# Complex-decay attention and two gated layers on one core: attention work spread over five positions of a slot

## The chip, the cores and the metric

The kernel runs on one core of one Trainium2 chip. Time is device microseconds of a whole execution. The engines are TensorE (PE in the profile), VectorE (DVE), ScalarE (ACT), GpSimd (POOL) and SyncE (SP), which issues most DMAs. Each engine works through its own program in order and waits for the others by semaphores.

## The reference

Three computations follow one another. The first is attention by a recurrence with complex decays, for 4 batches, 8 heads, 768 steps and a head width of 48:

```python
mag = np.sqrt(a_re * a_re + a_im * a_im)
scale = np.minimum(mag, 0.999) / (mag + 1e-06)
a_re_n, a_im_n = (a_re * scale, a_im * scale)
for t in range(S):
    new_re = ar * S_re - ai * S_im
    new_im = ar * S_im + ai * S_re
    S_re, S_im = (new_re + kv, new_im)          # kv = k_t outer v_t
    y[:, :, t] = np.einsum('bhd,bhde->bhe', q[:, :, t], S_re)
```

Its output, as 3072 tokens of 384 numbers, goes through `g = h * clip(h + 3, 0, 6) / 6; g @ w_out` with `h = x @ w_in` (384 to 2048 and back), and then through a second layer of the same sizes with `g = max(h, 0) + alpha * min(h, 0)`. All in float32.

## The kernel before

Attention is cut into 24 chunks of 128 steps (`NCH`), six to a batch, all heads at once. A chunk's decays become a magnitude part (`t_fb`: forward and backward running products, by scans on VectorE) and a phase part (`t_phase`, then `t_frac`, the turn without its whole part, then `t_trig`, cosine and sine on ScalarE). `prod` is q and k times these. Eight DMAs from SP and four from ScalarE's queue (`stack`) lay `prod` out by head in `st`. On TensorE then come `score` (two banks of four heads, `gp` and `yp`), `turn_k` (k transposed), `outputs` (masked scores times v, plus the carried state) and `new_state` (k times v, in `gp`). VectorE masks the scores (`mask`) and makes the next carried state `s_pad` (`state`); ScalarE copies the transposed k (`copy_k`).

The feed-forward layers work on units of 384 tokens, three chunks each. Every float32 operand is split in a high part and a low part, and each product takes three matmuls (`three`). An item n is one block of 128 hidden columns of one unit; 16 items make a unit. `hidden(n)` is nine matmuls of 384 columns from `x_parts` into one of two `hp` banks, `output(n)` nine into `op`. Between them lie the gate on ScalarE (`gate_of`), its product on VectorE (`gate1`), the high part on ScalarE (`high`) and the low part on GpSimd (`low`). TensorE runs `output(n)` and then `hidden(n + 3)`; the other engines work two items ahead (`n + 2`). At the end of a unit ScalarE copies `op` to `out_sb` (`leave`), and the next unit's first `output` waits for that (`o_left`). The second layer runs after all of the first; its items have no attention beside them.

The order of everything is written out by hand. `places()` yields slots s = -3 to 24 with five positions (six where a slot has six items). In a slot s the code handles four chunks at different ages: c0 = the slot's own chunk (scores to state), c1 = the next (angle, phases, products, stack), c2 (magnitude, clip, inverse, ratios), c3 (squares). Slot 3 has no chunk of its own, so chunks from 3 on sit in slot c + 1. Slots 3 to 6 have 3, 4, 3 and 4 items, from slot 7 on 5, 5, 6 in turn. The first `hidden` stands in slot 2. At each position an engine does its part of the item and then its pieces of attention work, in this order in the kernel before:

- VectorE (lines 819 to 853): position 0 `mags(c2)`, `phases(c1)`, `fractions(c1)`, both `mask(c0)`; position 1 `forward`, `backward`, `products` of c1; position 2 `x_low`, `state` of c0, `clip`, `numerators` of c2; position 3 two of three `inverse(c2)`; position 4 the third and `ratios(c2)`. `ratios` ends with a clamp of the tangent to 1.5 either way (line 686).
- ScalarE (lines 588 to 618): position 0 `angle(c1)`, `copy_k`; position 1 `waves(c1)`, `copy_k`, `magnitude(c2)`; position 2 `x_high(c0)` and, behind `high`, the four DMA issues of `stack(c1)`; position 4 `squares(c3)`. A weight split (`split_w`, line 567, its low half on GpSimd, line 471) stands at the end of a position: three each in slots -2 to 1, four each in slots 2 to 4 (`W_SPLITS`). A split waits for its piece of `wa_raw` or `wb_raw`.
- SP (lines 379 to 399): at position 2 `stack(c1)` behind `prod_done`, `spread(c0)` behind `x_done` (six DMAs inside `x_parts`, which hidden(16u) needs for all three chunks of unit u), the loads of `a` and of q and k; at position 3 the load of v and of weights.
- TensorE (lines 1061 to 1080): position 0 `score(c0, 0)`, `turn_k`, the item's output, `score(c0, 1)`, the item's hidden, `turn_k`; position 1 the item, `outputs`, `new_state`.

`score(c, 0)` writes the bank `gp` and waits for `state_ready` of the chunk before, which reads `gp`.

## Time and profile before

| | us |
|---|---|
| median of three runs (1093.77 to 1096.41) | 1095.03 |
| the profiled execution | 1091.72 |
| its span, first to last instruction | 1089.9 |
| PE busy | 971.5 |
| DVE busy | 700.0 |
| ACT busy | 487.9 |
| POOL busy | 304.5 |
| mean granted clock of TensorE | 0.986 |

The profile page cuts the span into 40 slices and lists groups of instructions by line; the trace can be asked for stretches, waits and single instructions. A wait line says which engine and line sat idle, for whom, for how long in total, how often and the longest. Starts of instructions are microseconds from the start of the span.

### The profile page before, as it was taken

Reading aid. Unit: us, or ns where it says so; the run is one execution under the profiler, and the core shown is the slowest. Engines: PE = TensorE matmul, PEld = TensorE weight load, DVE = VectorE, ACT = ScalarE, POOL = GpSimd, SP = SyncE. Lnnn points to the kernel's source line nnn. Section 1 sums busy time; section 2 is a strip of 40 time slices with the busy share of each in tenths; the row PEclk is TensorE's granted clock in tenths of the full one; section 3 lists DMA queues with packets and bytes.
Section 4 is the critical chain, followed back from the end, with each engine's and each line's share of the span. In section 5 each row is a group of like instructions: output and inputs, shape, how many; then the busy total and the mean of one; then the engine's idle time right before and its main releaser. Section 6 shows DMA issues by size and latency. Waiting matters only on the chain.

```text
span 1089.9 us, 16711 instructions
## 1 busy us (share of the span) xinstructions
PE 971.5 (89%) x6178; PEld 952.6 (87%) x6178; DVE 700.0 (64%) x1234; ACT 487.9 (45%) x814; POOL 304.5 (28%) x291
## 2 busy tenths in 40 slices
PE   0156698699999999999999999999999999999998
PEld 0156687699998898989999999999999999999998
DVE  1884899799898898998989224553334344343432
ACT  2553766556766666667665345321212221221211
POOL 1222431122222222222221233333333333333332
PEclk9999899899999999999999999999999999999999
DMA  8353223333342332333323360101101010101000
GB/s 164 101 156 75 68 71 77 85 97 75 95 103 69 93 82 82 97 87 91 93 56 82 94 221 1 45 1 44 35 11 44 1 45 1 44 1 44 1 23 23
DMA packets 84803, 72.84 MB, mean 67 GB/s; under 512 B 34928, under 2 KB 80496, under 8 KB 84336
## 3 DMA queue, kind: packets, MB, share of 16 engines
q1 hardware_dynamic: 75120, 63.43, 21.3%
q10 hardware_dynamic: 9600, 8.33, 3.0%
q8 instruction: 49, 0.80, 0.3%
q14 instruction: 34, 0.28, 0.1%
HBM read 40.90 MB, written 9.44 MB: 46 GB/s over the span
## 4 chain that ended last, share of the span: by engine, by line
PE 55%; DVE 19%; ACT 8%; SPq 7%; issue 6%; DMA 4%; ACTq 1%; DVEq 0%
PE hp L1023 9%; PE op L1023 9%; PE hp L1025 9%; PE hp L1024 9%; PE op L1025 9%; PE op L1024 8%; SPq L358 3%; DVE t_phase L693 3%; DVE t_fb L728 3%; SPq L350 2%; ACT L515 2%; DMA wa_raw<-w_in 2%; DVE scores L747 2%; DVE t_inv L677 2%; DVE gated L775 2%
## 5 line engine op out<-in xcount | busy, mean ns | idle before, releaser
L465 POOL TENSOR_TENSOR g_lo<-gated,g_hi 128x384 fp32r<-128x384 f32 x256 | 270.1, 1055 | 693.2 <-ACT g_hi L554 693.1
L554 ACT ACTIVATE g_hi<-gated 128x384 fp32r<-128x384 f32 x256 | 133.6, 522 | 357.7 <-DVE gated L789 291.4
L785 DVE TENSOR_SCALAR gate<-hp,alpha_sb 128x384 f32<-128x384 f32 x128 | 79.1, 618 | 230.5 <-PE hp L1025 230.5
L1023 PE MATMUL hp<-x_parts,wa_hi 128*128 128x384 f32 x384 | 133.9, 349 | 19.4 <-DMA x_parts<-x_parts 18.0
L1023 PE MATMUL op<-g_hi,wb_hi 128*128 128x384 f32 x384 | 136.7, 356 | 9.4 <-ACT out_sb L559 8.6
L547 ACT ACTIVATE gate<-hp,half 128x384 f32<-128x384 f32 x128 | 73.7, 576 | 134.0 <-PE hp L1025 91.7
L1025 PE MATMUL op<-g_hi,wb_lo 128*128 128x384 f32 x384 | 130.9, 341 | 0.0
L1024 PE MATMUL hp<-x_parts,wa_hi 128*128 128x384 f32 x384 | 130.9, 341 | 0.0
L1024 PE MATMUL op<-g_lo,wb_hi 128*128 128x384 f32 x384 | 130.7, 340 | 0.0
L1025 PE MATMUL hp<-x_parts,wa_lo 128*128 128x384 f32 x384 | 130.6, 340 | 0.0
L1023 PE MATMUL op<-g_hi,wa_hi 128*128 128x384 f32 x384 | 129.9, 338 | 0.7 <-issue 0.7
L1025 PE MATMUL op<-g_hi,wa_lo 128*128 128x384 f32 x384 | 129.8, 338 | 0.0
L1025 PE MATMUL hp<-x_parts,w2i_lo 128*128 128x384 f32 x384 | 129.5, 337 | 0.0
L1024 PE MATMUL hp<-x_parts,w2i_hi 128*128 128x384 f32 x384 | 129.2, 336 | 0.0
L1023 PE MATMUL hp<-x_parts,w2i_hi 128*128 128x384 f32 x384 | 129.0, 336 | 0.0
L1024 PE MATMUL op<-g_lo,wa_hi 128*128 128x384 f32 x384 | 128.8, 335 | 0.0
L775 DVE SCALAR_TENSOR_TENSOR gated<-gate,hp 128x384 f32<-128x384 f32 x128 | 69.5, 543 | 74.8 <-ACT gate L547 74.7
L986 PE MATMUL gp<-st 96*128 96x128 f32 x192 | 30.5, 310 | 72.4 <-DMA st<-prod 72.3
L1023 PEld LDWEIGHTS hp<-x_parts,wa_hi 128*128 128x128 f32 x384 | 73.9, 192 | 22.5 <-DMA x_parts<-x_parts 20.1
L986 PEld LDWEIGHTS gp<-st 96*128 96x128 f32 x192 | 28.7, 220 | 73.7 <-DMA st<-prod 73.7
L1023 PEld LDWEIGHTS op<-g_hi,wb_hi 128*128 128x128 f32 x384 | 73.7, 192 | 12.0 <-ACT out_sb L559 9.3
L789 DVE SCALAR_TENSOR_TENSOR gated<-hp,gate 128x384 f32<-128x384 f32 x128 | 71.4, 558 | 4.4
(97 smaller groups left out, 1877.0 us busy)
## 6 DMA issues: line engine op xcount, KB each, us to landing
st<-prod SPq DMA_DIRECT2D x48, 145.1 KB, 3.1
st<-prod ACTq DMA_DIRECT2D x48, 145.1 KB, 2.9
a_sb<-a_in SPq DMA_DIRECT2D x24, 288.0 KB, 3.4
qk_sb<-qk_in SPq DMA_DIRECT2D x24, 288.0 KB, 3.5
v_pad<-v_in SPq DMA_DIRECT2D x24, 192.0 KB, 3.4
x<-out_sb SPq DMA_DIRECT2D x8, 576.0 KB, 3.2
x_raw<-x SPq DMA_DIRECT2D x8, 576.0 KB, 4.6
out<-out_sb SPq DMA_DIRECT2D x8, 576.0 KB, 3.2
```

The costliest lines, as they stand in the source:

```text
L358: sp.dma_start(to, rows).then_inc(st_landed[c % 2], 16)
L465: pool.tensor_tensor(g_lo[:, at, :], gated[:, at * UT:(at + 1) * UT], g_hi[:, at, :].bitcast(F32), ALU.subtract).then_inc(glo_done, 1)
L547: act.activation(gate[:, n % 2 * UT:(n % 2 + 1) * UT], hp[:, n % 2, 0:UT], ACT.Relu, bias=half[:, 0:1], scale=1.0 / 6.0).then_inc(gate_don ...
L554: act.activation(g_hi[:, at, :], gated[:, at * UT:(at + 1) * UT], ACT.Copy).then_inc(ghi_done, 1)
L693: scan = dve.tensor_tensor_scan(t_phase[:, 0, k, :], ones[:, :], t_dt[:, 1, k, :], start, ALU.mult, ALU.add)
L775: dve.scalar_tensor_tensor(out=gated[:, to], in0=gate[:, at], scalar=1.0, in1=hp[:, n % 2, 0:UT], op0=ALU.min, op1=ALU.mult).then_inc(gate ...
L785: dve.tensor_scalar(gate[:, at], hp[:, n % 2, 0:UT], 0.0, alpha_sb[:, m:m + 1], ALU.min, ALU.mult).then_inc(gate_done, 1)
L789: dve.scalar_tensor_tensor(out=gated[:, to], in0=hp[:, n % 2, 0:UT], scalar=0.0, in1=gate[:, at], op0=ALU.max, op1=ALU.add).then_inc(gated ...
L986: mm = pe.matmul(score_banks[k][:, h % G4, :], st[:, c % 2, h, 1, 0:CH], st[:, c % 2, h, 0, 0:CH], start=True, stop=True)
L1023: pe.matmul(acc, lhs[0], rhs[0], start=start, stop=False)
L1024: pe.matmul(acc, lhs[0], rhs[1], start=False, stop=False)
L1025: return pe.matmul(acc, lhs[1], rhs[0], start=False, stop=stop)
```

## The change

The weight splits move to slots 0 to 4. The clamp and its semaphore go; ScalarE's arctangent waits for the ratios. On VectorE `forward` moves to position 0 ahead of `phases`; `fractions`, the masks and `backward` stand in position 1; a new piece `factors` (the copy into `prod` and the product with q and k, split off from `forward` and `backward`) and `products` in position 2; `x_low`, `clip`, `numerators` and one `inverse` in position 3; `state`, two `inverse` and `ratios` in position 4. On ScalarE `magnitude` moves from position 1 to 2 and `stack` from 2 to 3. On TensorE `score` and `turn_k` of one half stand in position 0 and of the other in position 1, `outputs` between the halves of position 2, `new_state` at the head of position 3; at a unit's first item the next hidden goes ahead of the output. `ones` is handed over as a slice of itself, which changes nothing. The diff, without those lines:

```diff
@@ -59,7 +59,7 @@
 NWI, NWP = WSZ // WPC, 2 * WSZ // WPC
 W_DMA = 1024
 W_LOADS = {-1: range(0, 2), 0: range(2, 4)}
-W_SPLITS = {-2: 3, -1: 3, 0: 3, 1: 3, 2: 4, 3: 4, 4: 4}
+W_SPLITS = {0: 5, 1: 5, 2: 5, 3: 4, 4: 5}
 ITEMS = {CPU: 3, CPU + 1: 4, CPU + 2: 3, CPU + 3: 4}
 NRP = 12
 RP = WSZ // NRP
...
@@ -511,7 +511,7 @@
                 act.activation(flat(t_ce, 1), flat(t_mag, 0), ACT.Identity, bias=tiny[:, 0:1]).then_inc(eps_set, 1)
 
             def angle(c):
-                act.wait_ge(clamp_done, c + 1)
+                act.wait_ge(ratio_done, c + 1)
                 act.activation(flat(t_dt, 1), flat(t_dt, 1), ACT.Arctan).then_inc(arctan_set, 1)
                 act.wait_ge(arctan_set, c + 1)
                 act.activation(flat(t_dt, 1), flat(t_dt, 1), ACT.Copy, scale=TURN).then_inc(angle_set, 1)
...
@@ -598,12 +598,11 @@
                     high(n + GSTEP)
                 if pos == 0 and keeps:
                     copy_k(c0, 0)
-                if pos == 1:
-                    if keeps:
-                        copy_k(c0, 1)
-                    if c2 is not None:
-                        magnitude(c2)
-                if pos == 2 and c1 is not None:
+                if pos == 1 and keeps:
+                    copy_k(c0, 1)
+                if pos == 2 and c2 is not None:
+                    magnitude(c2)
+                if pos == 3 and c1 is not None:
                     stack(c1)
                 if pos == 4 and c3 is not None:
                     squares(c3)
...
@@ -682,15 +681,13 @@
                 both = t_dt[:, :, :, :].rearrange("p x k t -> p x (k t)")
                 dve.tensor_tensor(both, both, flat(t_inv, 0).unsqueeze(1).to_broadcast([P, 2, KT_DM * CH]), ALU.mult
                                   ).then_inc(ratio_done, 1)
-                dve.wait_ge(ratio_done, c + 1)
-                dve.tensor_scalar(flat(t_dt, 1), flat(t_dt, 1), 1.5, -1.5, ALU.min, ALU.max).then_inc(clamp_done, 1)
 
             def phases(c):
                 dve.wait_ge(angle_set, c + 1)
                 need(dve, frac_done, c)
                 for k in range(KT_DM):
                     start = 0.0 if is_first(c) else t_frac[:, 0, k, CH - 1:CH]
-                    scan = dve.tensor_tensor_scan(t_phase[:, 0, k, :], ones[:, :], t_dt[:, 1, k, :], start,
+                    scan = dve.tensor_tensor_scan(t_phase[:, 0, k, :], ones, t_dt[:, 1, k, :], start,
                                                   ALU.mult, ALU.add)
                 scan.then_inc(phase_done, 1)
 
...
@@ -714,22 +711,25 @@
                 dve.tensor_scalar(end_inv[:, :], ends, DECAY_MIN, None, ALU.max).then_inc(end_step, 1)
                 dve.scalar_tensor_tensor(out=ok_all[:, :], in0=ends, scalar=DECAY_MIN, in1=ok_all[:, :],
                                          op0=ALU.is_ge, op1=ALU.min).then_inc(end_step, 1)
-
-                if c > 0:
-                    dve.wait_ge(st_landed[(c - 1) % 2], 16 * STACK_DMAS * ((c - 1) // 2 + 1))
-                dve.tensor_copy(prod[:, :, :, 0, CH], ends.unsqueeze(1).to_broadcast([P, 2, KT_DM])
-                                ).then_inc(end_step, 1)
                 dve.wait_ge(end_step, 4 * c + 1)
                 dve.reciprocal(t_fb[:, 1, :, CH - 1], end_inv[:, :]).then_inc(end_step, 1)
 
             def backward(c):
-                dve.wait_ge(end_step, 4 * c + 4)
+                dve.wait_ge(end_step, 4 * c + 3)
                 for k in range(KT_DM):
                     scan = dve.tensor_tensor_scan(t_fb[:, 1, k, CH - 2::-1], t_dt[:, 0, k, CH - 1:0:-1],
                                                   ones[:, 0:CH - 1], t_fb[:, 1, k, CH - 1:CH], ALU.mult, ALU.mult)
                 scan.then_inc(back_done, 1)
+
+            def factors(c):
+
+                if c > 0:
+                    dve.wait_ge(st_landed[(c - 1) % 2], 16 * STACK_DMAS * ((c - 1) // 2 + 1))
+                dve.tensor_copy(prod[:, :, :, 0, CH], t_fb[:, 0, :, CH - 1].unsqueeze(1).to_broadcast([P, 2, KT_DM])
+                                ).then_inc(end_step, 1)
                 dve.wait_ge(qk_landed, 48 * (c + 1))
                 dve.wait_ge(back_done, c + 1)
+                dve.wait_ge(end_step, 4 * c + 4)
                 every = lambda t: t[:, :, :, :].rearrange("p x k t -> p (x k t)")
                 dve.tensor_tensor(every(t_fb), every(t_fb), every(qk_sb), ALU.mult).then_inc(qb_done, 1)
 
...
@@ -821,33 +821,37 @@
                     if c2 is not None:
                         mags(c2)
                     if c1 is not None:
+                        forward(c1)
                         phases(c1)
+                if pos == 1:
+                    if c1 is not None:
                         fractions(c1)
                     if c0 is not None:
                         if c0 == 0:
                             dve.wait_ge(masks_set, 4)
                         mask(c0, 0)
                         mask(c0, 1)
-                if pos == 1 and c1 is not None:
+                    if c1 is not None:
+                        backward(c1)
+                if pos == 2 and c1 is not None:
                     if c1 == 0:
                         dve.wait_ge(pads_set, 3)
-                    forward(c1)
-                    backward(c1)
+                    factors(c1)
                     products(c1)
-                if pos == 2:
+                if pos == 3:
                     if c0 is not None:
                         x_low(c0)
-                        if not is_last(c0):
-                            state(c0)
                     if c2 is not None:
                         clip(c2)
                         numerators(c2)
-                if pos == 3 and c2 is not None:
-                    inverse(c2, 0)
-                    inverse(c2, 1)
-                if pos == 4 and c2 is not None:
-                    inverse(c2, 2)
-                    ratios(c2)
+                        inverse(c2, 0)
+                if pos == 4:
+                    if c0 is not None and not is_last(c0):
+                        state(c0)
+                    if c2 is not None:
+                        inverse(c2, 1)
+                        inverse(c2, 2)
+                        ratios(c2)
                 if s == CPU - 1 and pos == POSITIONS - 1:
                     for k in range(GSTEP):
                         gate1(k)
...
@@ -1058,31 +1062,39 @@
                                (g_hi[:, n % GRING, :], g_lo[:, n % GRING, :]), m == 0, m == MT_FF - 1)
                 mm.then_inc(o_done, 1)
 
+
+            def first_half(n):
+                if n % MT_FF == 0 and n + HSTEP < 2 * N1:
+                    hidden(n + HSTEP)
+                else:
+                    output(n)
+
+            def second_half(n):
+                if n % MT_FF == 0:
+                    output(n)
+                elif n + HSTEP < 2 * N1:
+                    hidden(n + HSTEP)
+
             for s, pos, n, c0, c1, c2, c3 in places():
                 keeps = c0 is not None and not is_last(c0)
-                if pos == 0 and c0 is not None:
-                    score(c0, 0)
+                if pos < 2 and c0 is not None:
+                    score(c0, pos)
                     if keeps:
-                        turn_k(c0, 0)
+                        turn_k(c0, pos)
                 if n is not None:
-                    output(n)
-                if pos == 0 and c0 is not None:
-                    score(c0, 1)
+                    first_half(n)
+                if pos == 2 and c0 is not None:
+                    outputs(c0)
+                if pos == 3 and keeps:
+                    new_state(c0)
                 if n is not None:
-                    hidden(n + HSTEP)
-                if pos == 0 and keeps:
-                    turn_k(c0, 1)
-                if pos == 1 and c0 is not None:
-                    outputs(c0)
-                    if keeps:
-                        new_state(c0)
-                if s == CPU - 1 and pos == 2:
+                    second_half(n)
+                if s == CPU - 1 and pos == 3:
                     for k in range(HSTEP):
                         hidden(k)
             for n in range(N_ATT, 2 * N1):
-                output(n)
-                if n + HSTEP < 2 * N1:
-                    hidden(n + HSTEP)
+                first_half(n)
+                second_half(n)
                 if n == N_ATT:
                     pe.wait_ge(bad_found, 1)
                     pe.matmul(gp[0:1, 0:KT_DM + 1], half[:, 0:1], bad[:, :], start=True, stop=True
```

## Rows read from the trace of the kernel before

**Rows 1.** Busy time by stretch: each engine's busy us (instructions), then clock, DMA share, GB/s.

```profile
202.00:606.00 404.00, 385.94 (x2752) 374.05 (x2752) 363.30 (x650) 261.45 (x431) 95.39 (x90) 0.99 0.33 85
```

**Rows 2.** Waits of TensorE over the span: total us, times, longest.

```profile
PE gp L986 <- DMA st<-prod: 72.3, 5, 48.9
PE hp L1023 <- DMA x_parts<-x_parts: 18.0, 7, 7.5
...
PE op L1023 <- ACT out_sb L559: 8.6, 6, 1.9
```

**Rows 3.** Timeline of ScalarE, 21 to 31 us: start, us, instruction, [idle before <-releaser].

```profile
21.00 0.63 ACT L567 ACTIVATE wa_hi<-wa_raw 128x512 fp32r<-128x512 f32 x1 [14.57 <-DMA wa_raw<-w_in]
...
22.94 0.52 ACT L507 ACTIVATE t_mag<-t_sq 128x384 f32<-128x384 f32 x1
...
30.20 0.63 ACT L567 ACTIVATE wa_hi<-wa_raw 128x512 fp32r<-128x512 f32 x1 [5.58 <-DMA wa_raw<-w_in]
```

**Rows 4.** Timeline of TensorE: the first hidden, two slot starts, two late hiddens.

```profile
104.23 0.69 PE L1023 MATMUL hp<-x_parts,wa_hi 128*128 128x384 f32 x1 [3.73 <-DMA x_parts<-x_parts]
...
343.77 0.45 PE L1023 MATMUL hp<-x_parts,wa_hi 128*128 128x384 f32 x1 [1.32 <-DMA x_parts<-x_parts]
...
369.86 1.05 PE L986 MATMUL gp<-st 96*128 96x128 f32 x8
...
391.51 1.06 PE L986 MATMUL gp<-st 96*128 96x128 f32 x8
...
416.77 0.58 PE L1023 MATMUL hp<-x_parts,wa_hi 128*128 128x384 f32 x1 [1.88 <-DMA x_parts<-x_parts]
...
417.48 0.52 PE L1025 MATMUL hp<-x_parts,wa_lo 128*128 128x384 f32 x1
```

**Rows 5.** Timeline of VectorE, one slot of five items and the next slot's fractions.

```profile
373.07 1.94 DVE L693 TENSOR_TENSOR_SCAN t_phase<-ones,t_frac,t_dt 128x128 f32<-128x128 f32 x3 [0.63 <-ACT t_dt L517]
375.04 0.36 DVE L700 TENSOR_SCALAR t_trig<-t_phase 128x384 f32<-128x384 f32 x1
...
377.11 0.55 DVE L775 SCALAR_TENSOR_TENSOR gated<-gate,hp 128x384 f32<-128x384 f32 x1
...
385.59 0.97 DVE L765 TENSOR_TENSOR s_pad<-s_sum,st 96x384 f32<-96x384 f32 x1
...
393.41 0.36 DVE L686 TENSOR_SCALAR t_dt<-t_dt 128x384 f32<-128x384 f32 x1
393.69 0.55 DVE L775 SCALAR_TENSOR_TENSOR gated<-gate,hp 128x384 f32<-128x384 f32 x1
...
397.50 0.36 DVE L700 TENSOR_SCALAR t_trig<-t_phase 128x384 f32<-128x384 f32 x1
```

**Rows 6.** Timeline of VectorE, before the first item.

```profile
41.32 1.83 DVE L740 TENSOR_TENSOR prod<-t_fb,t_trig 128x768 f32<-128x768 f32 x2
...
52.77 1.60 DVE L703 TENSOR_TENSOR t_frac<-t_phase,t_trig 128x384 f32<-128x384 f32 x1
...
77.48 1.83 DVE L740 TENSOR_TENSOR prod<-t_fb,t_trig 128x768 f32<-128x768 f32 x2
```

**Rows 7.** Timeline of SP's DMA issues, the stack of the same slot.

```profile
405.71 3.83 SPq L358 DMA_DIRECT2D st<-prod  x6
```

**Rows 8.** Timeline of GpSimd.

```profile
52.70 1.26 POOL L471 TENSOR_TENSOR wa_lo<-wa_raw,wa_hi 128x512 fp32r<-128x512 f32 x1 [4.74 <-ACT wa_hi L567]
```

**Rows 9.** Timeline of ScalarE, 398 to 410 us.

```profile
398.49 0.53 ACT L522 ACTIVATE t_trig<-t_frac 128x384 f32<-128x384 f32 x1 [0.91 <-DVE t_frac L703]
...
402.16 1.28 ACT L507 ACT_TABLE_LOAD   x1
...
404.54 0.57 ACT L547 ACTIVATE gate<-hp,half 128x384 f32<-128x384 f32 x1
...
406.99 2.88 ACTq L531 DMA_DIRECT2D st<-prod  x4
409.98 0.58 ACT L547 ACTIVATE gate<-hp,half 128x384 f32<-128x384 f32 x1 [2.47 <-issue]
```

More of the change, by code:

```diff
@@ L176, in build @@
         k_rows = sb("k_rows", [P, HEADS, ROWS2], F32, room)
-        ones = sb("ones", [P, CH], F32, room)
+        ones = sb("ones", [P, CH], F32, room)[:, :]
         causal = sb("causal", [P, CH], F32, room)
@@ L708, in forward @@
                 for k in range(KT_DM):
-                    scan = dve.tensor_tensor_scan(t_fb[:, 0, k, :], t_dt[:, 0, k, :], ones[:, :], 1.0,
+                    scan = dve.tensor_tensor_scan(t_fb[:, 0, k, :], t_dt[:, 0, k, :], ones, 1.0,
                                                   ALU.mult, ALU.mult)
@@ L812, in _ @@
             dve.memset(tiny[:, :], 1e-6).then_inc(consts_set, 1)
-            dve.memset(ones[:, :], 1.0)
+            dve.memset(ones, 1.0)
             dve.memset(worst_all[:, :], -1e30)
```

2 lines of the change are left out of this document (1 added, 1 removed).

## The prediction

> **What bounds the kernel now.** First the stages. From 202 to 606 us TensorE is busy 385.9 of 404 us [rows 1]; the stretch behind it, to the end, is dense feed-forward work whose order the change leaves as it was except at unit borders, where TensorE's waits show nothing [rows 2]. So the end comes earlier or later by what TensorE loses up to 606 us. The waits say where: 72.3 us on the landing of `st`, 48.9 of it before its first matmul, 18.0 on the spreading of `x_parts`, 8.6 on the copy of `out_sb` [rows 2]. The start is bound by ScalarE, which sits in front of a weight split waiting for `wa_raw` [rows 3] while the attention chain has nothing else to wait for. The middle, slots 7 to 23, I judge by slot length: between two slot starts with five items and no wait lie 391.51 - 369.86 = 21.65 us on TensorE [rows 4]. VectorE took 393.69 - 370.90, about 22.8 us, over the same slot with one wait of 0.63 us [rows 5]: it is as full as TensorE and falls behind in a short slot. A six-item slot is 3.12 us longer. The 17 slots from 202 to 606 us (twelve with five items, five with six) would so cost TensorE 383.7 us, and about 378 with the lighter first and last chunks of a batch. They took 404: 26 us is all that the middle can give back.
>
> **The start (gain).** With no splits in slots -2 and -1 nothing holds ScalarE there. The square root of the first chunk began at 22.94 us, behind a wait of 14.57 us [rows 3]; its input is ready at about 6.7 us, and with a table load of 1.28 us it begins at about 8. From there the first chunk's chain is VectorE's (from 22.94 to its products at 41.32 it takes 18.4 us with its waits now [rows 3, 6]) and loses the second wait of 5.58 us as well. The stack of chunk 0, its products starting at 41.32, starts its products at about 22; the gain there is 19.3. The third chunk's `a` rows now queue behind the weights, which end at 30.2 us as now [rows 3], so it lands at about 31 and takes 3 us of it back from VectorE, and the products of chunk 1 come 18.4 us earlier. Chunk 2's products start 77.48 now [rows 6]; by the same `qk` transfer they start 18.9 earlier. From there to the first `hidden`, which starts 104.23 [rows 4], nothing shortens: stack, spread and `v` leave SP in one line behind the products. Five splits a slot instead of three cost some: while one ran on GpSimd (52.70 to 53.96) a subtraction on VectorE took 1.60 us and not 0.56 [rows 8, 6]; four more in slots 0 and 1, of which one in four meets such an operation, 1 us. Sum -18. Bounds: -20.2 (both waits of rows 3), and -12 if the landing of the third chunk's `a` and of the first stack slips by another 6.
> The Trainium skill ("SBUF — State Buffer", section SBUF: two separate sides) says that the port pair which VectorE and GpSimd share is an exclusive lock held for a whole instruction. The rows just named agree in kind. By that rule alone all four further splits could block VectorE for their 1.26 us each, and the start would gain 13 in place of 18.
>
> **The middle, what gets longer.** One gate stands at the head of each position on ScalarE and VectorE, and both run in order. So a position of VectorE cannot start before ScalarE has come to its own gate of the same number. Now VectorE does its longest piece (scans, products) between two gates and ScalarE hides behind it; the change cuts it in the middle. Follow one slot:
> Fractions to position 2. ScalarE's `waves` starts 1.0 us after VectorE starts the fractions (397.50 to 398.49), and its next free moment, behind waves, g_hi and the k copy, is 402.16 [rows 5, 9]: 4.66 us after. The gate for position 2 stands there, and VectorE can use it 0.6 us later (5.3). Meanwhile VectorE has the rest of the fractions, two masks and the backward scans: from 375.04 to 377.11, and 2.05 or, without GpSimd beside it, 1.3 us of scans, 3.4 to 4.1 together. It stands idle for 1.2 to 1.9 us.
> Position 2 to 3. ScalarE now has x_high, g_hi and then the magnitude (404.54 - 402.16 = 2.4 us [rows 9]) ahead of its gate; VectorE is idle for another 0.6.
> Position 3 to 4. The four DMA issues of `stack` hold ScalarE from 406.99 to 409.98 [rows 9], 3.0 us; they now lie ahead of the gate of position 4. Idle 0.6. Behind that gate stands `state` (about 1.5 us), which in the kernel before lies in position 2 (385.6 to 386.5 its last part [rows 5]).
> VectorE's work itself shrinks by the clamp, 393.69 - 393.41 = 0.28 us [rows 5], and by the wait of `phases` for the angle, 0.63 [rows 5], which `forward` now covers; and a scan pair that met GpSimd may miss it (1.5). It is 20.4 to 21.9 us of work plus 3.1 of idling: 23.3 to 24 a slot against TensorE's 21.65.
> Who waits: `score` of the next chunk needs `state`, since both use the bank `gp`. In the kernel before `state` is ready at 386.5, 5 us before the next slot at 391.51 [rows 4, 5]; now it comes at 22.4 to 23.3 us after the slot's start. TensorE waits for 0.8 us in the slot after a six-item one and for 1.65 in the next, nothing in the six-item one. Over 17 slots, with the lighter first and last chunks: +13 (bounds 0, if state fits in, and +20).
> Second, the spread. In six-item slots `hidden` of the next unit stands at the end of its own slot and waits for the last chunk's spread, 1.88 us at 416.77 [rows 4], 6.8 us in five such slots. From the first product to that `hidden` SP needs 11.06 us (405.71 to 416.77 [rows 7, 4]). VectorE enters the slot 3.0 us behind TensorE in place of about 2.2 and takes 12.7 us to the first product in place of 12.0, so each wait grows by 1.5 to 3.5: +13 for five (bounds +3, +17). Where TensorE waited for 1.88 us its matmuls then took 0.52 us [rows 4] in place of the 0.34 that is usual on the page, at the low one of the two clock levels (1.2 GHz), for nine matmuls, and 1.5 us more were lost; two more such places, +3.
>
> **The middle, what gets shorter.** At a unit's first item `hidden` and `outputs` now stand ahead of the `output` that needs the emptied `op` banks; 1.5 us or more cover the copy, so the 8.6 us [rows 2] go, and with them the cold matmuls behind the longer two of these waits, 2.5 as I size them: -11. Sum of slots 7 to 23: 13 + 13 + 3 - 11 = +18. Bounds -14 and +26.
> In slots 3 to 6 there are three or four items, TensorE is slack and the same chain sets the pace: the gate of position 1 waits for TensorE's first item where fractions and masks went ahead of it, and then comes the 5.3 us above. Slot by slot +1.5, +1.5, +1.5 and +2.8 to the first product; four clamps and angle waits less are in it. I count +6 (bounds -3 and +8). What `state`, `v` and the weights load behind slot 24 has 10 us of slack and costs nothing.
>
> **Sum.** On the profiled execution, 1091.7 us: -18 + 6 + 18 = +6, 1098. The runs' median is 3.3 above that execution, so 1101 against 1095.0.
> The Trainium skill ("ScalarE: Activation LUTs", section What ACT_TABLE_LOAD costs) gives a switch of tables as 1283 ns and a drain of 1380 ns. The trace shows the 1.28 us, and from the load at 402.16 to the gate at 404.54, with two activations between, 2.4 us [rows 9], which leaves no room for a drain; with the drain ScalarE's stretch from fractions to the gate of position 2 would be 1.4 us longer, and the middle some 10 us dearer.
>
> **Rivals.**
> R1, the balance works: VectorE's idling of 3.1 us a slot does not come, because the positions are as even as they look, and of the 26 us of the middle the 11 above go. For it: five gates and 22 us of work fit 21.65. Against it: ScalarE's row of 4.66 us behind the fractions. -18 at the start, -11 in the middle, 0 in slots 3 to 6: 1066. 10%.
> R2, start only: the lengthened chain is paid by the slack of six-item slots, no more than the out_sb copies give back; slots 3 to 6 +3. 1095 - 18 + 3 = 1080. For it: VectorE also lags by 1.2 a slot today and recovers. Against: `state` now sits behind the lag. 17%.
> R3, more clocks lost: the waits of 1.65 us at slot starts also drop the clock. An idle time of 1.32 us at 343.77 did not, 1.88 at 416.77 did [rows 4]; eleven slots by 1.5: 1117. It decides somewhere between these two lengths. 10%.
> R4, the start gives back half: the first stack and `a` queue behind the weights for 6 to 9 us longer, with the middle as forecast: 1109. Against: all weights have landed at 30.2 us. 10%.
> Forecast: the start's gain is eaten by the in-order chain from fractions over ScalarE to `state`: 53%, own range 1091 to 1112. It decides at +18: if slots 3 to 23 lose less than that, in place of the 24 I count, the change is a gain.
>
> **Chances.** A measurement of this kernel tells 0.2%, 2.2 us, from no change (1092.8 to 1097.2). Faster: R1, R2 and a sixth of the forecast, 36%. Same: 10 of the forecast's 53 and 2 of R4's, 12%. Slower: the rest, 52%. The range: 1078 to 1114; it leaves out R1 and most of R3.
>
> **What would show it.** Start: the first square root at about 8 us and the first `hidden` of `hp` near 86 us. Middle: TensorE's waits get a new row, `gp` of the score line waiting for `s_pad` of the state line, over 8 us in total; the row of `out_sb` is gone; the `x_parts` row stays above 15 us; VectorE idles ahead of its gates, some 3 us a slot. Slots of five items are 22.5 to 23.5 us long. Wrong, if they are 21.7 us and no such row is there: then R1 or R2. Wrong at the start, if the first `hidden` is not before 92 us.

## The result, and the profile after it

The changed kernel takes 1107.1 us (median of four runs, 1106.6 to 1108.4) against 1094.4 for the kernel before; the ratio is 1.0115, 95% interval 1.0097 to 1.0132. It is slower by 12.7 us, where 1101 with a range of 1078 to 1114 was forecast. The profiled execution took 1106.7 us, its span 1105.0 (before: 1091.7 and 1089.9).

The end of each stage, read off TensorE's timeline, splits the 15.1 us between the two spans (in us, each figure rounded by itself):

| stage | before | after | difference | forecast |
|---|---|---|---|---|
| start, to the first `hidden` | 104.2 | 90.2 | -14.0 | -18 |
| slots 3 to 6, to the score of slot 7 | 97.8 | 106.5 | +8.8 | +6 |
| slots 7 to 23, to the score of slot 24 | 403.7 | 425.2 | +21.5 | +18 |
| the rest | 484.2 | 483.1 | -1.1 | 0 |

TensorE's waits over the span (total us, times, longest), kernel after:

```profile
PE gp L990 <- DMA st<-prod: 68.9, 8, 35.8
PE hp L1027 <- DMA x_parts<-x_parts: 33.7, 7, 8.9
PE gp L990 <- DVE s_pad L765: 13.4, 9, 4.1
...
PE op L1027 <- ACT out_sb L559: 0.3, 1, 0.3
```

Against [rows 2]: the longest wait for `st` is 13.1 us shorter, yet the row as a whole only 3.4; the spread (`x_parts`) has nearly doubled; a row for `s_pad`, which is the state of the recurrence, is new; the `out_sb` row is all but gone.

VectorE's and ScalarE's waits on each other over the span, kernel after; in the kernel before the first row was 74.7 us in 45 waits and the second 13.3 in 10:

```profile
DVE gated L775 <- ACT gate L547: 134.6, 65, 5.4
```

```profile
ACT t_trig L522 <- DVE t_frac L700: 58.7, 23, 3.6
```

The stretch that answers to [rows 1], slots 7 to 23, kernel after (busy us of PE, PEld, DVE, ACT, POOL with instructions, then clock, DMA share, GB/s):

```profile
196.70:621.90 425.20, 392.33 (x2750) 379.69 (x2749) 349.80 (x634) 260.05 (x431) 104.56 (x90) 0.97 0.31 81
```

It holds practically the same matmuls (2750 and 2752), and they are busy 6.4 us longer at a mean granted clock of 0.97 where it was 0.99. TensorE idles 32.9 us in it, against 18.1. VectorE's busy time fell by 13.5 us and that bought nothing.

TensorE's timeline at the first `hidden`, at two slot starts, and at the `hidden` that ends a six-item slot, kernel after (these answer to [rows 4]; start, us, instruction, [idle before <-releaser]):

```profile
90.20 0.69 PE L1027 MATMUL hp<-x_parts,wa_hi 128*128 128x384 f32 x1 [4.97 <-DMA x_parts<-x_parts]
...
371.26 1.16 PE L990 MATMUL gp<-st 96*128 96x128 f32 x8 [0.99 <-DMA st<-prod]
...
394.31 1.13 PE L990 MATMUL gp<-st 96*128 96x128 f32 x8 [1.13 <-DVE s_pad L765]
...
421.55 0.69 PE L1027 MATMUL hp<-x_parts,wa_hi 128*128 128x384 f32 x1 [3.77 <-DMA x_parts<-x_parts]
...
424.28 0.52 PE L1029 MATMUL hp<-x_parts,wa_lo 128*128 128x384 f32 x1
```

394.31 - 371.26 = 23.05 us, where the same slot took 21.65. In slots 7 to 23 those of five items take 22.4 to 24.4 us (the last 22.0), those of six 28.6 to 30.3; before it was 21.6 to 24.4 and 25.8 to 28.2.

### The profile page after: what moved, and what is told of

Its sections match the earlier page's. It is cut to its first block, busy times and chain, and to the rows that moved or that the text cites. A ratio compares the mean times of both kernels' runs of the same rounds, so it can differ in the third digit from the quotient of the medians.

```text
span 1105.0 us, 16686 instructions
## 1 busy us (share of the span) xinstructions
PE 975.5 (88%) x6178; PEld 957.3 (87%) x6178; DVE 684.8 (62%) x1210; ACT 486.3 (44%) x814; POOL 315.3 (29%) x291
## 4 chain that ended last, share of the span: by engine, by line
PE 54%; DVE 19%; issue 8%; SPq 8%; ACT 6%; DMA 3%; ACTq 1%; DVEq 0%
PE hp L1027 9%; PE hp L1029 8%; PE hp L1028 8%; PE op L1027 8%; PE op L1029 8%; PE op L1028 8%; SPq L358 4%; DVE gated L775 3%; DVE t_inv L676 2%; SPq L350 2%; DVE prod L740 2%; DVE t_fb L706 2%; DVE t_fb L734 2%; PE gp L990 2%; DMA st<-prod 2%
## 5 line engine op out<-in xcount | busy, mean ns | idle before, releaser
L465 POOL TENSOR_TENSOR g_lo<-gated,g_hi 128x384 fp32r<-128x384 f32 x256 | 280.6, 1096 | 705.2 <-ACT g_hi L554 705.2
L1027 PE MATMUL hp<-x_parts,wa_hi 128*128 128x384 f32 x384 | 136.0, 354 | 33.7 <-DMA x_parts<-x_parts 33.7
L1028 PE MATMUL hp<-x_parts,wa_hi 128*128 128x384 f32 x384 | 131.9, 343 | 0.0
L990 PE MATMUL gp<-st 96*128 96x128 f32 x192 | 35.6, 344 | 82.4 <-DMA st<-prod 68.9
L1027 PEld LDWEIGHTS hp<-x_parts,wa_hi 128*128 128x128 f32 x384 | 74.6, 194 | 38.3 <-DMA x_parts<-x_parts 35.7
L990 PEld LDWEIGHTS gp<-st 96*128 96x128 f32 x192 | 32.2, 249 | 87.0 <-DMA st<-prod 85.4
L1028 PEld LDWEIGHTS hp<-x_parts,wa_hi 128*128 128x128 f32 x384 | 74.8, 195 | 0.0
```

What stands on the lines that cost most here:

```text
L465: pool.tensor_tensor(g_lo[:, at, :], gated[:, at * UT:(at + 1) * UT], g_hi[:, at, :].bitcast(F32), ALU.subtract).then_inc(glo_done, 1)
L990: mm = pe.matmul(score_banks[k][:, h % G4, :], st[:, c % 2, h, 1, 0:CH], st[:, c % 2, h, 0, 0:CH], start=True, stop=True)
L1027: pe.matmul(acc, lhs[0], rhs[0], start=start, stop=False)
L1028: pe.matmul(acc, lhs[0], rhs[1], start=False, stop=False)
```

## How the slot runs now

VectorE over this slot, kernel after (answers to [rows 5]):

```profile
378.73 0.35 DVE L697 TENSOR_SCALAR t_trig<-t_phase 128x384 f32<-128x384 f32 x1
...
380.79 1.22 DVE L720 TENSOR_TENSOR_SCAN t_fb<-t_dt,t_fb,ones 128x127 f32<-128x127 f32 x3
383.87 0.56 DVE L775 SCALAR_TENSOR_TENSOR gated<-gate,hp 128x384 f32<-128x384 f32 x1 [1.86 <-ACT gate L547]
...
385.71 2.45 DVE L740 TENSOR_TENSOR prod<-t_fb,t_trig 128x768 f32<-128x768 f32 x2
388.08 0.54 DVE L775 SCALAR_TENSOR_TENSOR gated<-gate,hp 128x384 f32<-128x384 f32 x1
...
389.61 1.37 DVE L666 TENSOR_TENSOR t_inv<-t_ce,a_sb 128x384 f32<-128x384 f32 x1
...
392.63 0.49 DVE L775 SCALAR_TENSOR_TENSOR gated<-gate,hp 128x384 f32<-128x384 f32 x1
...
393.61 0.55 DVE L765 TENSOR_TENSOR s_pad<-s_sum,st 96x384 f32<-96x384 f32 x1
```

ScalarE over the same stretch, kernel after (answers to [rows 9]; ACTq are its DMA issues):

```profile
379.71 0.53 ACT L522 ACTIVATE t_trig<-t_frac 128x384 f32<-128x384 f32 x1 [3.16 <-DVE t_frac L700]
380.26 1.28 ACT L523 ACT_TABLE_LOAD   x1
381.55 0.52 ACT L523 ACTIVATE t_trig<-t_frac 128x384 f32<-128x384 f32 x1
...
383.27 0.57 ACT L547 ACTIVATE gate<-hp,half 128x384 f32<-128x384 f32 x1
...
387.38 0.56 ACT L547 ACTIVATE gate<-hp,half 128x384 f32<-128x384 f32 x1
...
388.66 2.69 ACTq L531 DMA_DIRECT2D st<-prod  x4
391.46 0.58 ACT L547 ACTIVATE gate<-hp,half 128x384 f32<-128x384 f32 x1 [2.27 <-issue]
```

Read the two together. The fractions start at 378.73. ScalarE has been idle for 3.16 us waiting for them, does its waves, and reaches the gate of position 2 at 383.27; VectorE runs out of work at 382.0 and starts behind that gate at 383.87, 5.14 us after the fractions (5.3 forecast). First ScalarE waits for VectorE and then VectorE for ScalarE, within one slot. That pair of waits was laid open by splitting VectorE's long position. At this gate 1.48 to 1.86 us stand in every slot from 7 on but a unit's first, and there 2.87 or 2.88. The state is written at 394.16, 22.9 us after the slot's start, and the score of the next chunk follows at 394.31.

GpSimd in that slot, kernel after:

```profile
385.06 1.41 POOL L465 TENSOR_TENSOR g_lo<-gated,g_hi 128x384 fp32r<-128x384 f32 x1 [1.00 <-ACT g_hi L554]
389.26 1.30 POOL L465 TENSOR_TENSOR g_lo<-gated,g_hi 128x384 fp32r<-128x384 f32 x1 [2.79 <-ACT g_hi L554]
```

The first product runs beside the first of them. Over the whole kernel the products' group says the same, 969 ns in the mean before and here 1266. (Other operations lost such a neighbour by the change; the last section has the balance.)

```profile
L740 DVE TENSOR_TENSOR prod<-t_fb,t_trig 128x768 f32<-128x768 f32 x48 | 58.8, 1266 | 3.4 <-ACT t_trig L525 0.6 <-DVE t_fb L734 0.5
```

## The experiments

Times are medians beside runs of the kernel before on the same chip (1094.0 to 1094.3), ratios are to that kernel with 95% intervals. P0 to P4 are the five positions.

**Undoing and isolating parts.** The split counts alone, put on the kernel before:

```diff
-W_SPLITS = {-2: 3, -1: 3, 0: 3, 1: 3, 2: 4, 3: 4, 4: 4}
+W_SPLITS = {0: 5, 1: 5, 2: 5, 3: 4, 4: 5}
```

> The kernel before with the new places of the weight splits alone. Theory C (in-order chain: the gate at the head of each position makes VectorE and ScalarE take turns, from the fractions over the waves to the state): the start's gain of the change, 14.0 us to the first hidden, comes alone, and the middle stays as before, so 1094.4 - 14 = 1080, slots of 21.65 us where nothing waits. Theory P (it is the order on TensorE that costs): the same here. Theory S (the five splits a slot disturb slots 0 to 4 and cost part of the middle): 1084 or more.

Measured 1084.2, ratio 0.9911 (0.9881 to 0.9940), with the first `hidden` at 92.14 us (104.23 before) and slots much as before. The gain of the start is real, 10 us in the medians, and it is the splits that bring it. C's 1080 was missed all the same, and the median lies on the line of S (1084 or more). The profiled execution, a quick one of 1080.0 us, wins 12.1 us to the first `hidden`, loses 1.7 in slots 3 to 6 and wins 1.4 in slots 7 to 23, so that a cost of the kind S names is not excluded. R2 was right about the part and wrong about the whole.

The converse, the kernel after with the old split counts (the same two lines, exchanged):

> The kernel after with the split counts of before, so only the three orders and the clamp are new. The parts add (theory): the splits alone gave 10 us on the kernel before, and the start of the kernel after is 14 us shorter, so this kernel comes to 1117 to 1121, with the first hidden near 104 us and slots as in the kernel after (22.4 to 24.4 us). Rival: the splits moved into slots 0 to 2 cost the new order something (VectorE is met by GpSimd in positions that have no slack): then the loss without them is under 7 us, 1114 or less.

Measured 1120.1, ratio 1.0235 (1.0212 to 1.0258); from slot 7 on slots of five items take 22.7 to 24.4 us (the last 22.1). The parts add: without the splits everything else of the change costs 26 us, and the splits are worth 13.0 us here and 10.0 on the kernel before. The first `hidden` came at 102.12, so that 12 us of the start's 14 belong to the splits and 2 to the rest of the change.

Only the border, on the kernel before: at a unit's first item `hidden` goes ahead of `output`.

```diff
+            def first_half(n):
+                if n % MT_FF == 0 and n + HSTEP < 2 * N1:
+                    hidden(n + HSTEP)
+                else:
+                    output(n)
...
-                    output(n)
+                    first_half(n)
...
-                    hidden(n + HSTEP)
+                    second_half(n)
```

> The kernel before with one edit: at a unit's first item hidden goes ahead of output. Theory C: the 8.6 us of TensorE's wait for out_sb go, and with them the matmuls at 1.2 GHz behind the longer of those waits, about 2.5: 1083. Rival D (what is saved at a border is lost at the next spread, since VectorE sets the slots): 1090 or more, and the x_parts waits grow by what the out_sb waits lose.

Measured 1087.3 over ten runs, ratio 0.9940 (0.9920 to 0.9960): between the two. TensorE's waits of that kernel:

```profile
PE gp L986 <- DMA st<-prod: 75.9, 7, 49.8
PE hp L1023 <- DMA x_parts<-x_parts: 19.6, 7, 7.9
PE yp L1006 <- issue: 12.1, 9, 4.9
```

The `out_sb` row of 8.6 us [rows 2] has shrunk to 0.3, but the waits for `x_parts` have grown by 1.6, those for `st` by 3.6 and those of the last row by 2.3, and the score of slot 24 comes at 604.4 us, only 1.3 before its old time. (The two profiled executions, 1089.1 and 1091.7 us, lie 2.6 apart where the medians lie 6.7 apart, so the rows show less than the whole gain.) In these rows most of what TensorE no longer waits for `out_sb` it waits for something else. The term of -11 was too large by 4 in the medians; that VectorE's pace takes the rest back is argued from the rows.

The three parts that carry no new order of attention work (splits, border, clamp gone) together on the kernel before; of the clamp:

```diff
-                dve.wait_ge(ratio_done, c + 1)
-                dve.tensor_scalar(flat(t_dt, 1), flat(t_dt, 1), 1.5, -1.5, ALU.min, ALU.max).then_inc(clamp_done, 1)
```

> The kernel before with the three parts of the change that are not the spreading: weight splits placed as changed, hidden ahead of output at unit borders, no clamp. Theory C: they add up, 10 (measured for the splits alone) + 11 + about 3 (24 clamps of 0.28 us, half of them on the path): 1070 to 1076. Rival D: 1080 or more.

Measured 1075.5, ratio 0.9833 (0.9796 to 0.9870), in C's range. The new positions of the attention work are therefore what costs: 1107.1 - 1075.5 = 31.6 us (30.9 by the two ratios).

**Which engine's order is it?** The kernel after with TensorE's places of before (both score pairs in P0, `outputs` and `new_state` in P1):

```diff
-                if pos < 2 and c0 is not None:
-                    score(c0, pos)
+                if pos == 0 and c0 is not None:
+                    score(c0, 0)
...
-                if pos == 2 and c0 is not None:
-                    outputs(c0)
-                if pos == 3 and keeps:
-                    new_state(c0)
...
+                if pos == 1 and c0 is not None:
+                    outputs(c0)
+                    if keeps:
+                        new_state(c0)
```

> The changed kernel with TensorE's attention pieces at the places of the kernel before (both scores in position 0, outputs and new_state at the end of position 1), hidden ahead of output at unit borders kept; VectorE and ScalarE as changed. Theory C: the chain does not run over TensorE, 1104 to 1110; outputs in position 1 may even wait for the masks, which now stand in VectorE's position 1: up to +5. Theory P: 15 us or more better, 1092 or less.

Measured 1113.8, ratio 1.0171 (1.0134 to 1.0208): dearer than the change. TensorE's later places are not the cause; put back, `outputs` meets masks that VectorE has not finished, and `new_state` waits another 9.9 us in 17 waits for ScalarE's copy of k:

```profile
PE yp L1010 <- DVE scores L747: 10.4, 11, 1.4
```

With ScalarE's places of before (magnitude in P1, stack in P2):

```diff
-                if pos == 2 and c2 is not None:
-                    magnitude(c2)
-                if pos == 3 and c1 is not None:
+                if pos == 1:
...
+                    if c2 is not None:
+                        magnitude(c2)
+                if pos == 2 and c1 is not None:
                     stack(c1)
```

> The changed kernel with ScalarE's positions as in the kernel before (magnitude in position 1, stack in 2), VectorE and TensorE as changed. Theory C: the gate of position 2 stands 2.4 us later behind the fractions, the gate of 4 no longer behind the stack: the chain from fractions to state is the same work in another order or longer, so 1105 to 1125 and VectorE's idle time ahead of its gates grows. Theory P: 1107 unchanged within 3. If the places of ScalarE's pieces, and not VectorE's, were at fault, it would fall under 1095.

A miss: 1203.9, ratio 1.0995 (1.0965 to 1.1025), where 1105 to 1125 was expected. VectorE now makes the products in P2, so a stack in P2 holds ScalarE, and with it the gates of P3 and P4, until they are done. Of one slot, VectorE at the gates of P2 and P3 and ScalarE at that of P3:

```profile
439.52 0.55 DVE L776 SCALAR_TENSOR_TENSOR gated<-gate,hp 128x384 f32<-128x384 f32 x1 [4.34 <-ACT gate L547]
...
447.42 0.55 DVE L776 SCALAR_TENSOR_TENSOR gated<-gate,hp 128x384 f32<-128x384 f32 x1 [3.63 <-ACT gate L547]
```

```profile
446.81 0.58 ACT L547 ACTIVATE gate<-hp,half 128x384 f32<-128x384 f32 x1 [6.18 <-issue]
```

The first of these waits was 1.86 in the kernel after; what it has grown by (2.5 us) is the magnitude, which ScalarE now does ahead of that gate. The other is the stack's. I had weighed the first and not the second, and this run moves both at once. Slots take 28 to 32 us:

```profile
PE gp L991 <- DVE s_pad L766: 33.7, 9, 10.5
```

With VectorE's places of before (P0 phases and fractions, P1 scans and products, P2 `x_low`, state and numerators, P3 and P4 the inverses):

```diff
                     if c1 is not None:
-                        forward(c1)
                         phases(c1)
-                if pos == 1:
-                    if c1 is not None:
                         fractions(c1)
...
-                if pos == 2 and c1 is not None:
+                if pos == 1 and c1 is not None:
...
+                    forward(c1)
+                    backward(c1)
                     factors(c1)
                     products(c1)
-                if pos == 3:
+                if pos == 2:
```

> The changed kernel with VectorE's positions as in the kernel before (forward, backward, factors and products in position 1, masks and fractions in position 0, state in 2), ScalarE and TensorE as changed. Theory C: VectorE no longer waits for the gate of position 2 in the middle of its piece, and state is ready early: 1107 - 20 to 28 us, 1079 to 1087, and TensorE's wait for s_pad under 2 us in total. Theory P: no more than 5 us better than 1107.

A miss: 1143.5, ratio 1.0468 (1.0421 to 1.0515), where 1079 to 1087 was expected. TensorE at two slot starts, VectorE and ScalarE in the slots before them, of this kernel:

```profile
389.63 1.16 PE L987 MATMUL gp<-st 96*128 96x128 f32 x8 [2.53 <-DMA st<-prod]
...
417.81 1.46 PE L987 MATMUL gp<-st 96*128 96x128 f32 x8 [4.12 <-DMA st<-prod]
```

```profile
408.38 0.55 DVE L763 TENSOR_TENSOR s_sum<-gp,s_pad 96x384 f32<-96x384 f32 x1 [2.25 <-PE gp L1019]
```

```profile
385.24 2.87 ACTq L531 DMA_DIRECT2D st<-prod  x4
```

The products end at 379.8, but ScalarE, still in the order of the kernel after, issues its half of the stack at 385.24 behind the gate of P3, 5.5 us later, so the stack lands late for the score at 389.63. And VectorE's state in P2 waits for `new_state`, which TensorE does in P3: 25.2 us in slots 7 to 23, as 12 waits. I had counted what VectorE would no longer wait for and not what the two others, left as they were, would now do too late for it. What follows: the three orders fit each other only as a set, and giving one engine its old order back costs 7 to 97 us more. To find the costly step, small pieces have to move so that each still meets its partners.

**Moving single pieces of the kernel after.** The state from P4 into P3, right behind `x_low`:

```diff
                         x_low(c0)
+                        if not is_last(c0):
+                            state(c0)
...
-                    if c0 is not None and not is_last(c0):
-                        state(c0)
```

> The changed kernel with state back ahead of the gate of position 4 (in position 3, behind x_low). Theory C: TensorE's wait for s_pad (13.4 us) goes, but the turns of VectorE and ScalarE still need 23.3 us a slot, so the time comes back as later stacks and spreads: the waits for st and x_parts grow by about half of it, 1100 to 1105. Rival H (the wait for state is the whole cause): 1107 - 13.4 - 1.5 for each clock loss behind it, 1094 or less.

Measured 1102.3, ratio 1.0073 (1.0045 to 1.0101): 4.8 us better than the change, as C said. The `s_pad` row is gone, but the score, no longer waiting for the state, often waits for the stack instead (`st` in 17 waits, 8 in the kernel after):

```profile
PE gp L990 <- DMA st<-prod: 81.8, 17, 36.2
PE hp L1027 <- DMA x_parts<-x_parts: 29.7, 7, 8.9
```

What TensorE gained is in the row of the spread (33.7 us in the kernel after). One more thing changed with this move: the state now stands between `x_low` and `clip`, and L666 behind it meets GpSimd only seldom (in the kernel after it took 1208 ns in the mean):

```profile
L666 DVE TENSOR_TENSOR t_inv<-t_ce,a_sb 128x384 f32<-128x384 f32 x24 | 15.5, 647 | 0.2
```

So the 4.8 us may come from the earlier state or from VectorE's shorter work (13.5 us in that group, 6.5 over all groups); this run cannot tell them apart.

The fractions at the end of P0, ahead of the gate of P1, so that ScalarE gets them while VectorE has the rest of its work to do:

```diff
                         phases(c1)
+                        fractions(c1)
                 if pos == 1:
-                    if c1 is not None:
-                        fractions(c1)
```

> The changed kernel with the fractions moved from the head of VectorE's position 1 to the end of its position 0, ahead of one gate. Theory C: the waves on ScalarE start 0.5 us or more earlier against VectorE's masks and scans, which now have the gate, masks and scans to fill the stretch: VectorE's idle time ahead of the gate of position 2 (1.86 us a slot) falls by about 0.5 to 1.3, and each slot of five items by as much: 1085 to 1097. Rival G (the slots are set by VectorE's work and GpSimd's port, not by the turns): no change, 1104 to 1110.

Measured 1099.3 over ten runs, ratio 1.0047 (1.0026 to 1.0069), 7.8 us better than the change and 2.3 above C's range. VectorE's wait at the gate of P2 fell from 1.86 to 1.39 us in an ordinary slot and from 2.88 to 2.42 in a unit's first. The late fractions, the first link of the forecast chain, are the larger of the two pieces tried. Both moves:

> The changed kernel with both moves: fractions at the end of position 0 and state behind x_low in position 3. Theory C: the two links lie on one chain and each shortens it by its own length; 8 us and 5 us measured alone, together 10 to 14: 1093 to 1097, and TensorE's waits for st and x_parts fall with it. Theory H (state alone): no better than the better of the two, 1099.

Measured 1096.4, ratio 1.0013 (0.9986 to 1.0040): back at the time of the kernel before. Two moved calls undo 10.7 of the 31.6 us; that the second adds to the first is not shown, since the interval of the fractions alone overlaps with this one. The waits for `st` did not fall as expected (79.4 us over the span, 68.9 in the kernel after); those for the spread did (26.9, 33.7 after). The remaining 21 were not taken apart. From 200 us to the end of the slots TensorE waits 15.6 us on the spread and 8.0 on `st` in this kernel, against 7.2 and none in the one with the three parts, which is 16 of them, and the stack leaves a position later than there. That points at the products and the stack in P2 and P3, but was not tried by itself.

**A better version.** From the kernel of the three parts, `forward` ahead of `phases` (the reordering of the change that fills the wait for the angle, the 0.63 us of [rows 5]):

```diff
+                        forward(c1)
                         phases(c1)
                         fractions(c1)
...
-                    forward(c1)
                     backward(c1)
```

> The three parts on the kernel before (splits, border, no clamp), and on VectorE forward ahead of phases in position 0, the one piece of the spreading that covers a wait (the angle, 11.6 us in 16 slots). Theory C: VectorE sets the slots now, so the wait goes on the path in slots without other waits: 1075.5 - 5 to 8. Rival G: the longer position 0 delays the masks and the gate of 1 by what it saves, 1074 to 1077.

Measured 1069.9, ratio 0.9781 (0.9725 to 0.9838), in C's range; its runs (1066.8 to 1071.1) all lie below those of the three parts (1075.3 to 1076.6). The wait for the angle is gone, and the products meet GpSimd here as in the kernel after:

```profile
L738 DVE TENSOR_TENSOR prod<-t_fb,t_trig 128x768 f32<-128x768 f32 x48 | 58.4, 1256 | 3.3 <-ACT t_trig L525 1.0
```

So the longer products alone do not make a slow kernel. And on top of it, on SP, the spread ahead of the stack for a unit's last chunk:

```diff
+                    ahead = c0 is not None and c0 >= CPU and c0 % CPU == CPU - 1
+                    if ahead:
+                        spread(c0)
                     if c1 is not None:
                         stack(c1)
-                    if c0 is not None:
+                    if c0 is not None and not ahead:
                         spread(c0)
```

> The kernel of e10_fwd0, and on SP in every third slot (the last chunk of a unit) the spread ahead of the next chunk's stack. Theory C: the stack's 5.15 us of issues no longer stand ahead of the spread; five waits for x_parts of 1 to 2 us go, with one or two losses of clock, and the stack lands 5 us later, 1 us too late for the next slot's score: 3 us better than e10_fwd0. Rival: the later stack costs more than the spread gives, 2 us or more worse than e10_fwd0, with a new wait for st of 2 us or more a unit.

Measured 1067.3, ratio 0.9779 (0.9717 to 0.9842), which can't be told from the one before it. TensorE's waits, first without and then with that move:

```profile
PE gp L984 <- DMA st<-prod: 63.4, 9, 38.2
PE hp L1021 <- DMA x_parts<-x_parts: 13.6, 5, 6.3
```

```profile
PE gp L987 <- DMA st<-prod: 67.8, 13, 36.3
PE hp L1024 <- DMA x_parts<-x_parts: 6.9, 2, 3.7
```

The spread's waits fell by 6.7 us and the stack's rose by 4.4: SP issues its DMAs one behind another (six in 3.83 us [rows 7]), and most of what one transfer gained there the next one lost.

## Why the prediction was right

The verdict and the mechanism held: the start's gain is eaten by the in-order chain from fractions over ScalarE to the state. The 1107.1 lie in the forecast's own range, 6 above its figure; the loss is twice the forecast one (+12.7 for +6), because the three terms missed by 2.8 to 4.0 us, all the same way. Experiments show that the new positions cost 31.6 us and that moving two links of the chain gives 10.7 of them back; the rest of the chain is read off the traces. Step by step:

**The start: -18 forecast, -14.0 measured.** The square root began at 7.46 us (about 8 forecast), and chunk 0's products started at 20.89 in place of 41.32 (-20.4; 19.3 forecast). The step that failed is that "the products of chunk 1 come 18.4 us earlier". ScalarE and VectorE at the start, kernel after:

```profile
31.15 0.84 ACT L501 ACTIVATE t_sq<-a_sb 128x768 f32<-128x768 f32 x1 [7.81 <-DMA a_sb<-a_in]
...
33.72 0.52 ACT L515 ACTIVATE t_dt<-t_dt 128x384 f32<-128x384 f32 x1
```

```profile
43.44 2.83 DVE L740 TENSOR_TENSOR prod<-t_fb,t_trig 128x768 f32<-128x768 f32 x2
...
47.26 1.61 DVE L666 TENSOR_TENSOR t_inv<-t_ce,a_sb 128x384 f32<-128x384 f32 x1
...
55.16 2.21 DVE L690 TENSOR_TENSOR_SCAN t_phase<-ones,t_frac,t_dt 128x128 f32<-128x128 f32 x3
...
62.24 2.92 DVE L740 TENSOR_TENSOR prod<-t_fb,t_trig 128x768 f32<-128x768 f32 x2
```

```profile
43.32 1.26 POOL L471 TENSOR_TENSOR wa_lo<-wa_raw,wa_hi 128x512 fp32r<-128x512 f32 x1 [2.37 <-ACT wa_hi L567]
...
62.22 1.26 POOL L471 TENSOR_TENSOR wa_lo<-wa_raw,wa_hi 128x512 fp32r<-128x512 f32 x1 [5.14 <-ACT wa_hi L567]
```

The third chunk's `a` landed at 31.15, as forecast, but what it held up was the second chunk: its angle (33.72) stands on ScalarE behind the third chunk's squares. The second chunk's products started at 43.44 (59.40 before), 16.0 us earlier. Then the splits: I let one in four meet an operation of VectorE, and of those that ran from 43 to 64 us four did, at about 1.0 us each (the product pair 1.83 [rows 6] to 2.83 and 2.92; L666 0.56 to 1.61; the scans 1.2 to 2.21). In the kernel before one did between the second and the third chunk's products, at 0.6 us. The gain was 15.2 at the third chunk's products and 14.0 at the first `hidden`. The Trainium skill ("SBUF — State Buffer", section SBUF: two separate sides) has VectorE wait out the whole GpSimd instruction where that one started first; the 1.00 and 1.09 us lost on the two product pairs, beside splits of 1.26 us that began 0.12 and 0.02 us ahead of them, come near it. My 13 us by that rule counted the splits twice, with my own 1 us still in it; it should have been 14. That this is the measured figure is luck in good part: the landing took 2.4 us of the missing 4, which the rule has nothing to do with.

**Slots 3 to 6: +6 forecast, +8.8 measured.** Here VectorE's state sets a score already: that of slot 5 waits 4.1 us for it, the longest of the `s_pad` row, and slot 4, which ends there, became 3.5 us longer where I had 1.5. From the first `hidden` to slot 4 it was 2.8 (1.5 forecast).

**Slots 7 to 23: +18 forecast, +21.5 measured.** The waits came out as counted: state and stack at the slot starts 12.6 us (9.3 and 3.3; forecast +13, for the state alone), the spread +13.0 (6.8 to 19.8; forecast +13), `out_sb` -8.3 (forecast -8.6). TensorE's smaller waits fell by 2.5, so that it idled 14.8 us more. What was too small is the clock. I had 3 us for two more losses against 2.5 won back, a net of 0.5. TensorE's busy time rose by 6.4. From the end of slot 6 on it lost its high clock in seven places. In the four where `hidden` waited 3.8 us or more for the spread (8.9 at the end of slot 6, then 4.8, 3.8 and 4.9), it ran on at 0.52 us a matmul for eight or nine, the lower of the two clock levels (1.2 GHz), where 0.34 is usual. Behind the two waits of 3.2 us it began at 0.34, and the clock fell about 1 us later, over two or three of its matmuls and the eight of the score (1.91 us, elsewhere 1.13). The one left followed a wait for the stack (R3 below). The kernel before had four such places, two of them behind `out_sb`. The border alone, for which I had -11, gave 6.7 us in the medians and 1.4 in slots 7 to 23 of its profiled execution; its separate size in the changed kernel was not measured.

**The chain's links.** Fractions to position 2: 5.14 us (5.3), idle 1.86 (1.2 to 1.9). State 22.9 us after the slot's start (22.4 to 23.3). But the two idle times of 0.6 us ahead of positions 3 and 4 did not appear in this slot: the gates at 388.08 and 392.63 follow without a gap. In their place VectorE's work was longer, the products 2.45 us for 1.83 and L666 1.37 for 0.56, each beside one of the GpSimd rows above. ScalarE's gates at 387.38 and 391.46 would have held VectorE there had it been quicker, so the two causes cover each other. The idling ahead of gates, from 200 to 606 us, is 62.1 us in 29 waits against 24.5 in 17 before: 3.7 us a slot, that of position 2 and a further 3.1 to 5.4 behind each six-item slot.

**The rivals.** R1 (the balance works) fell by the slots of 23 us. R2 (start only) fell by the new `s_pad` row. R3 (the short waits at slot starts also drop the clock) happened once, behind 1.56 us at 522.86, where nine matmuls of 0.52 followed; behind 1.71 us at 243.68 and nine shorter ones it did not. R4 (half the start given back) is the nearest on the start, with another cause. And the drain behind a table load, cited from the Trainium skill ("ScalarE: Activation LUTs", What ACT_TABLE_LOAD costs), is not there: the load at 380.26 ends at 381.54 and the next activation starts at 381.55. Nor is it ahead of the load, since the activation before it ends at 380.24.

## What to carry to other kernels

Where several in-order engines meet at one gate per step, even shares of work are no measure: follow each producer to its consumer over the gates, put first in its step whatever another engine waits for, and let the long step stand where it hides the other engine's latency (this last is read from the traces and was not tried alone). Change such orders in small pieces that still meet their partners, not an engine at a time. Measure the parts of a bundle singly: here three good parts (-18.5 us together) hid behind one bad one (+31.6), and in that one again `forward` in position 0 was good (some 6 us on the kernel of the three parts).

## What the runs showed of the hardware that I had not expected

- A wait of TensorE does not by its length alone decide the clock. In the kernel before, 1.94 us at one unit border (503.81) were followed by matmuls of 0.34 us and 1.92 us at another (215.38) by ten of 0.52:

```profile
215.38 0.57 PE L1023 MATMUL op<-g_hi,wb_hi 128*128 128x384 f32 x1 [1.92 <-ACT out_sb L559]
...
503.81 0.44 PE L1023 MATMUL op<-g_hi,wb_hi 128*128 128x384 f32 x1 [1.94 <-ACT out_sb L559]
```

After the change 1.71 us cost nothing and 1.56 us nine slow matmuls. Nine of them start 0.32 us apart in place of 0.17, so such a place costs 1.3 us. And the fall can come after the work has begun again, as behind the two waits of 3.2 us.
- Where an operation of VectorE stands in the slot decides whether it runs beside one of GpSimd, and each place is good for one operation and bad for another. Over the 24 chunks the change made three groups longer, the products by 14.3 us (58.8 against 44.5), L666 by 11.6 (29.0 against 17.4) and the forward scans by 10.0 (35.2 against 25.2), and two shorter, the backward scans by 14.1 (29.3 against 43.4) and the scans of the phases by 9.2 (36.9 against 46.1). Moving the state alone into position 3 took L666 down to 15.5. That the slot's order of gates is what brings the two engines together at the products is argued from the one slot shown, not tested.
- Four DMA issues on ScalarE take 2.69 us at 388.66 here and 2.88 in [rows 9] (up to 3.5 in other slots), and they hold its next activation for that time, and through the gate behind it the other engines too. Which step of the slot they stand in, together with the magnitude, which moved with them, was worth up to 97 us (1203.9 against 1107.1).
